# A retention, routing and GLU kernel: attention products turned round, first routing round without GpSimd arithmetic, TensorE rounds written out

## What is computed

```python
# retention over B=4 batches, H=8 heads, S=768 steps, D=64
state = gamma * state + k[t] (outer) v[t];   y[t] = q[t] @ state / sqrt(D)
x = y.transpose(0, 2, 1, 3).reshape(3072, 512)
# routing: 8 experts, 384 tokens each; all 3072*8 logits are taken in falling order,
# a token goes to the first expert that still has room
logits = x @ w_gate;  assigned = greedy(logits, cap=384)
out[e] = relu(x[e] @ w1[e]) @ w2[e]          # 512 -> 1024 -> 512
# gated unit on all tokens, d_ff = 1536
return (sigmoid(out @ w_gate2) * (out @ w_val)) @ w_out
```

## Time and profile before

| | us |
|---|---|
| three runs | 1206.94, 1212.17, 1213.2 (median 1212.17) |
| the profiled execution | 1207.1, its span 1205.4 |
| attention, to the first instruction of the search | 0 to 191.6 |
| first search and gather | 191.6 to 253.4 |
| eight rounds of work | 253.4 to 1194.2 |
| last copies and scatter | 1194.2 to 1205.4 |

### The profile page before, as it was taken

The page is one execution under the profiler, slowest core; times in us unless marked ns, Lnnn a source line. Parts: engine busy times, 40 slices in busy tenths (PEclk is TensorE's granted clock), DMA queues, the critical chain, the costliest instruction groups (busy, mean ns, idle before and its releaser), DMA issues.

```text
span 1205.4 us, 20115 instructions
## 1 busy us (share of the span) xinstructions
PE 1117.8 (93%) x7224; PEld 1032.8 (86%) x7224; DVE 573.7 (48%) x1423; ACT 339.7 (28%) x635; POOL 377.4 (31%) x365
## 2 busy tenths in 40 slices
PE   6999994169999999999999999999999999999996
PEld 6999993169889988998899889988998899899995
DVE  2343335865644564456345735572557255722111
ACT  2223222124123322332233223322331233223211
POOL 4432323245032513341234123322432143215200
PEclk9999996569999999999999999999999999999998
DMA  9878714223122211221132113111312131204100
GB/s 211 189 169 181 163 50 122 78 62 98 36 62 78 87 44 52 87 78 44 52 96 70 44 52 96 70 52 44 108 57 64 32 113 52 78 17 132 35 1 27
DMA packets 172925, 95.89 MB, mean 80 GB/s; under 512 B 80224, under 2 KB 158048, under 8 KB 172896
## 3 DMA queue, kind: packets, MB, share of 16 engines
q1 hardware_dynamic: 169056, 82.92, 26.2%
q0 software_dynamic: 3840, 12.59, 3.6%
HBM read 82.90 MB, written 12.58 MB: 79 GB/s over the span
## 4 chain that ended last, share of the span: by engine, by line
PE 68%; DVE 12%; issue 3%; ACT 1%; POOL 0%; DVEq 0%; POOLq 0%
PE bank L1103 18%; PE bank L1105 17%; PE bank L1104 17%; PE bank L1181 5%; PE bank L1183 5%; PE bank L1182 5%; DVE onehot L945 3%; DVE above L848 2%; DVE digit_f L868 1%; PE bank L1062 1%; PE bank L1098 1%; ACT ph L780 1%; PE bank L1070 1%; DVE pf L987 1%; DVE prefix L888 1%
## 5 line engine op out<-in xcount | busy, mean ns | idle before, releaser
L712 POOL TENSOR_TENSOR ring<-ring_raw,ring 128x512 fp32r<-128x512 f32 x192 | 247.4, 1296 | 456.2 <-ACT ring L760 451.9
L1103 PE MATMUL bank<-h2h,resident 128*128 128x384 f32 x768 | 263.3, 343 | 0.2
L1105 PE MATMUL bank<-h2h,resident 128*128 128x384 f32 x768 | 258.0, 336 | 0.0
L1104 PE MATMUL bank<-h2l,resident 128*128 128x384 f32 x768 | 257.6, 335 | 0.0
L987 DVE TENSOR_TENSOR pf<-bank,gate 128x384 f32<-128x384 f32 x96 | 53.2, 555 | 201.3 <-PE bank L1105 197.7
L1103 PEld LDWEIGHTS bank<-h2h,resident 128*128 128x128 f32 x768 | 144.4, 188 | 4.0 <-DVE h2l L978 0.4
L1104 PEld LDWEIGHTS bank<-h2l,resident 128*128 128x128 f32 x768 | 144.3, 188 | 3.2
L1105 PEld LDWEIGHTS bank<-h2h,resident 128*128 128x128 f32 x768 | 144.1, 188 | 0.0
L760 ACT ACTIVATE ring<-ring_raw 128x512 fp32r<-128x512 f32 x192 | 117.6, 623 | 70.6 <-DMA ring_raw<-in_moe_w_out_dram 40.9
L780 ACT ACTIVATE ph<-pf 128x384 fp32r<-128x384 f32 x96 | 50.4, 525 | 251.8 <-DVE pf L987 251.8
L776 ACT ACTIVATE gate<-bank 128x384 f32<-128x384 f32 x96 | 47.1, 491 | 212.0 <-PE bank L1105 212.0
(11 more groups left out here) (167 smaller groups left out, 1851.8 us busy)
## 6 DMA issues: line engine op xcount, KB each, us to landing
ring_raw<-in_moe_w_dram SPq DMA_DIRECT2D x128, 256.0 KB, 2.9
ring_raw<-in_moe_w_out_dram SPq DMA_DIRECT2D x64, 256.0 KB, 2.8
qraw<-in_q_dram SPq DMA_DIRECT2D x24, 256.0 KB, 3.6
kraw<-in_k_dram SPq DMA_DIRECT2D x24, 256.0 KB, 4.2
vraw<-in_v_dram SPq DMA_DIRECT2D x24, 256.0 KB, 4.7
xrows<-xrow SPq DMA_DIRECT2D x24, 256.0 KB, 2.2
resident_raw<-in_moe_w_gate_dram SPq DMA_DIRECT2D x12, 256.0 KB, 4.6
resident_raw<-in_moe_w_val_dram SPq DMA_DIRECT2D x12, 256.0 KB, 4.7
```

The costliest lines, as they stand in the source:

```text
L712: nc.gpsimd.tensor_tensor(ring[:, s, 1, :], ring_raw[s][:, :], ring[:, s, 0, :].bitcast(F32), ALU.subtract).then_inc(piece_lo, 1)
L1103: nc.tensor.matmul(ps, wh, xhi, start=start, stop=False)
L1104: nc.tensor.matmul(ps, wh, xlo, start=False, stop=False)
L1105: return nc.tensor.matmul(ps, wl, xhi, start=False, stop=stop)
```

## The change

It does six things.

- Attention on TensorE: y comes out transposed (`ps_y` holds features by tokens): `state` or `vraw` is the stationary operand with 64 columns, `qT` or `att` the moving one with 128, and the output goes to the half of the partitions that belongs to the head. The state's update is likewise one product a head, 64 columns of weights and 64 moving columns. The scores alternate between even and odd heads instead of four even ones and then four odd ones. `xTa` is now copied straight from `ps_y`, and the rows for HBM (`xrow`) from the transposed `ps_x`; the logits follow in the slot of those transposes, so there is one slot fewer.
- The first search: GpSimd no longer makes the 12 late low parts there, nor the first 8 of the ring. VectorE makes those 8 (`first_low`), four ahead of `x_low` and four behind it. The 12 late ones go into GpSimd's round 0, two after each of the pieces 16 to 21.
- GpSimd's round 0 stands ahead of its loop.
- TensorE's rounds are written out one after another, with no loop.
- `PART_GAP` is us(4).
- The last `out_products` counts each third (`rows_done`), and `out_rows` waits third by third.

```diff
-        DIGIT_GAP, LATE_GAP, PART_GAP = us(6.8), us(5), us(2)
+        DIGIT_GAP, LATE_GAP, PART_GAP = us(6.8), us(5), us(4)
...
# ScalarE, attention
-                        nc.scalar.activation(xTa[:, cc % 2, :, :], ps_x[:, :].rearrange("p (a t) -> p a t", a=KD),
-                                             ACT.Copy).then_inc(xT_ready, 1)
+                        nc.scalar.activation(xrow[:, cc, :], ps_x[:, :], ACT.Copy).then_inc(xrow_ready, 1)
...
-                        nc.scalar.activation(xrow[:, cc, :], ps_y[:, :], ACT.Copy, scale=SCALE).then_inc(xrow_ready, 1)
+                        nc.scalar.activation(xTa[:, cc % 2, :, :], ps_y[:, :].rearrange("p (a t) -> p a t", a=KD),
+                                             ACT.Copy, scale=SCALE).then_inc(xT_ready, 1)
...
# TensorE, attention
                         for a in range(KD):
-                            last = nc.tensor.transpose(ps_x[:, a * P:(a + 1) * P], xrow[:, cc, a * P:(a + 1) * P], ident[:, :])
+                            last = nc.tensor.transpose(ps_x[:, a * P:(a + 1) * P], xTa[:, cc % 2, a, :], ident[:, :])
...
                             if cc > 0:
-                                nc.tensor.matmul(ps_y[:, a * P:(a + 1) * P], qT[:, cc % 3, a, :], state[:, cc % 2, a, :],
-                                                 start=True, stop=False)
-                            for h in (2 * a, 2 * a + 1):
-                                last = nc.tensor.matmul(ps_y[:, h * D:(h + 1) * D], att[:, cc % 2, h, :], vraw[:, cc, h, :],
-                                                        start=cc == 0, stop=cc == 0 or h % 2 == 1)
+                                for half in range(2):
+                                    rows = slice(half * D, half * D + D)
+                                    nc.tensor.matmul(ps_y[rows, a * P:(a + 1) * P], state[:, cc % 2, a, rows], qT[:, cc % 3, a, :],
+                                                     start=True, stop=False)
+                            for half in range(2):
+                                rows = slice(half * D, half * D + D)
+                                last = nc.tensor.matmul(ps_y[rows, a * P:(a + 1) * P], vraw[:, cc, 2 * a + half, :],
+                                                        att[:, cc % 2, 2 * a + half, :], start=cc == 0, stop=True)
...
                             for a in range(NPAIR):
-                                last = nc.tensor.matmul(ps_u[:, a * P:(a + 1) * P],
-                                                        ks[:, cc, 2 * a:2 * a + 2, :].rearrange("p h d -> p (h d)"),
-                                                        vraw[:, cc, 2 * a:2 * a + 2, :].rearrange("p h d -> p (h d)"),
-                                                        start=True, stop=True)
+                                for half in range(2):
+                                    rows = slice(half * D, half * D + D)
+                                    last = nc.tensor.matmul(ps_u[rows, a * P + half * D:a * P + half * D + D],
+                                                            ks[:, cc, 2 * a + half, :], vraw[:, cc, 2 * a + half, :],
+                                                            start=True, stop=True)
...
-                        for half in range(2):
-                            rows = slice(half * D, half * D + D)
-                            if s is None or s - 2 >= 1:
-                                pe.wait_ge(att_ready, 2 * (u - 1) + half + 1)
-                            for a in range(NPAIR):
+                        if s is None or s - 2 >= 1:
+                            pe.wait_ge(att_ready, 2 * u)
+                        for a in range(NPAIR):
+                            for half in range(2):
+                                rows = slice(half * D, half * D + D)
                                 last = nc.tensor.matmul(ps_s[half][:, a * P:(a + 1) * P], kT[rows, cc % 2, a, :],
                                                         qT[rows, cc % 3, a, :], start=True, stop=True)
...
# GpSimd, second block
                     piece_low(i, n)
+                    if n >= 2 * RING:
+                        for k in late[:2]:
+                            late_low(k)
+                        late = late[2:]
...
-            for k in range(LATE):
-                late_low(k)
             gather(0)
-            for n in range(RING):
-                piece_low(0, n)
-            with pool.Fori(0, E - 1) as i:
-                one_round(i, True)
-            one_round(E - 1, False)
+            pool.wait_ge(piece_lo, RING)
+            one_round(0, True, list(range(LATE)))
+            with pool.Fori(1, E - 1) as i:
+                one_round(i, True, [])
+            one_round(E - 1, False, [])
...
# VectorE
+            def first_low(n):
+                dve.wait_ge(piece_hi, n + 1)
+                nc.vector.tensor_tensor(ring[:, n, 1, :], ring_raw[n][:, :], ring[:, n, 0, :].bitcast(F32),
+                                        ALU.subtract).then_inc(piece_lo, 1)
+
             def out_rows(i):
-                dve.wait_ge(out_done, KG * (i + 1))
                 for j in range(TT):
+                    dve.wait_ge(rows_done, TT * i + j + 1)
...
+            for n in range(RING // 2):
+                first_low(n)
             for a in range(KD):
                 x_low(0, a)
+            for n in range(RING // 2, RING):
+                first_low(n)
...
# TensorE, second block
-                        if j == TT - 1:
+                        if f == KG - 1:
+                            last.then_inc(rows_done, 1)
+                        elif j == TT - 1:
                             last.then_inc(out_done, 1)
...
-            with pe.Fori(0, E - 1) as i:
-                one_round(i, True)
-            one_round(E - 1, False)
+            for i in range(E):
+                one_round(i, i < E - 1)
```

More of the change, by code:

```diff
@@ L240, in retention_moe_glu_kernel @@
         out_done = sem("out_done")
+        rows_done = sem("rows_done")
         orow_ready = sem("orow_ready")
@@ L516, in body @@
                                                 ALU.mult).then_inc(qs_ready, 1)
-                    if alive(s, 5):
-                        bb, cc = unit(b, c, 5)
+                    if alive(s, 4):
+                        bb, cc = unit(b, c, 4)
                         u = bb * C + cc
@@ L548, in body @@
                                 causal[:, :].unsqueeze(1).to_broadcast([P, NPAIR, P]), ALU.mult).then_inc(att_ready, 1)
-                slots(dve, body, 0, U + 4)
+                slots(dve, body, 0, U + 3)
             @block.tensor
@@ L626, in body @@
                         pe.wait_ge(kT_ready, u + 1)
[L627 to L631 removed]
+                        if s is None or s - 2 >= 1:
[3 more added lines that the diff above has]
+                                rows = slice(half * D, half * D + D)
                                 last = nc.tensor.matmul(ps_s[half][:, a * P:(a + 1) * P], kT[rows, cc % 2, a, :],
                                                         qT[rows, cc % 3, a, :], start=True, stop=True)
[L634 to L636 removed]
+                                if a == NPAIR - 1:
+                                    last.then_inc(scores_done, 1)
+                slots(pe, body, 0, U + 3)
         block = ctx.enter_context(nc.Block())
@@ L725, in scatter, with one_round @@
                 pool.sem_inc(orow_free, 1)
-            def one_round(i, follows):
+            def one_round(i, follows, late):
                 gathered = not follows
```

26 lines of the change are left out of this document (10 added, 16 removed).

## The result

| | before | after |
|---|---|---|
| median of four runs | 1212.35 us | 1145.47 us |
| lowest and highest | 1206.94, 1213.2 | 1142.82, 1147.63 |
| profiled execution, its span | 1207.1, 1205.4 | 1147.63, 1145.9 |
| ratio of the times | | 0.9456 (95%: 0.9421 to 0.9491) |

The kernel is 5.4% faster. Split at the same events, the two profiled executions give this. The expert's rounds are measured from one set of x transposes to the next.

A forecast was written before the change was run, and what follows sets the result against it. TensorE's queue bounds attention, VectorE's chain the search, then dense TensorE with two waits a round. 29.1 + 14.3 - 2.5 + 11.3 + 1.4 = 53.6 us off 1207.1 or 1212.2 gives 1153.5 or 1158.6; forecast 1156, own range 1142 to 1166, overall 1140 to 1180.

The forecast's parts named there:

- Attention: First block, TensorE's queue: 1.24 us less a slot over 22 slots, 29.1 us in the sum, other ends included.
- y: Attention's output products: 32 instructions for 24, column halves side by side, 0.89 us gained a slot; one after another, 0.90 lost.
- update: State update in attention: 16 instructions of 64 by 64 for 8, taken as no change; range gain 0.45, loss 0.9.
- seams: Changes of how the array is cut in a slot: three instead of two, costing 0.20 us, between 0 and 0.4.
- The search: First search, GpSimd silent: comparisons faster, 7.3 us, and TensorE's first expert matmul no longer held by `digit_f`, 7.0; 14.3 us gained.
- Round 0: First expert round: 12 late GpSimd pieces slow VectorE's search there; 2.5 us lost, bounds 0 and 7.3.
- fourth rival: Expert rounds: TensorE's waits before L1089 and L1181 only move, and round 0 costs its 7.3 us; 1168 us, chance 0.10.
- The parts further apart: Expert rounds, PART_GAP at 4 us: 6.8 us of one-hot waits and 4.5 before L1181 go; 11.3, bounds 4 and 14.3.
- Loop and thirds: TensorE's written-out rounds and GpSimd's peeled round gain nothing; scatters at the end, started by thirds, gain 1.4 us.
- halves of columns don't overlap: Rival in attention's y: column halves run one after the other, +0.40 us a slot, total gain 15; 1194 us, chance 0.13.
- each change of half drains: Rival in attention: every switch between column halves in y and update costs 0.19 us, 97 lost; 1282 us, chance 0.04.
- loads come late: Rival in attention: later store and fuller DMA queues hold the slot at 6.6 us, 14 us lost; 1170 us, chance 0.08.

## Why the prediction came out right, and which terms were off

It said 1156 us, 1140 to 1180; the kernel takes 1145.5. The forecast, not a rival, is what happened, but the sum was 6 us too small by the profiled executions, and two of its terms erred in opposite directions.

**Attention** gave 40.0 us where the sum had 29.1. By the full slot, predicted 7.57 to 6.33 and measured 5.70:

| us a full slot | predicted | measured | from |
|---|---|---|---|
| scores | -0.55 | -0.55 | 1.64 to 1.09 |
| y | -0.89 | -0.99 | 2.68 to 1.69 |
| update | 0 (bound -0.45) | -0.42 | 1.09 to 0.67 |
| seams | +0.20 | +0.10 | 2.16 to 2.25 |

The mechanism was right for the scores and for y, whose halves do overlap, and one more seam came, at half its price. The mis-sized term is the update, and with it the cause that was taken to set a step. The prediction had the bound at the right place (0.45) and took the other value, arguing that loads of 128 columns cost 0.112 us with 64 or with 128 moving columns, so that the weights' columns set the step. In the runs 64 columns of weights take 0.11 us a pair with 128 moving columns (y) and 0.058 with 64 (the update, 16 loads in 0.60 us: in the trace its pairs start at 98.03, 98.14, 98.19, 98.25 and so on). Both old rows and new ones fit a step set by the larger of the two; that is a fit to four combinations, not a test. In the earlier trace rows the larger was 128 everywhere, so those rows could not tell one from the other; what would have was to ask which of the two numbers had ever been seen alone. The update's 0.42 us are worth 7.7 over the some 18 slots that have one, and with the cut kept the same from y on, no seam came between y and the update. The tenth in y and the tenth in the seams make 4.4 us more over 22 slots. That is 12.1 us; the sum was exceeded by 10.9, so 1.2 went at the two ends of attention. Of that 1.1 is a wait that the kernel before doesn't have, of TensorE for GpSimd's `ks` at 23.01 us.

**The search** gave 14.0 against 14.3. That comparisons go back to 1.03 us, that `digit_f` was held up and not slow, and that `first_low` hides behind `xh`, all came as worked out; the first expert matmul comes 47.8 us behind the search's start, 47.5 expected.

**Round 0** cost more than the 2.5 us taken. Alone, the change of the search lengthens it by 5.3 to 7.2 us (123.63 against 118.30 and 116.39 in kernels with the old search). In the kernel after it is 124.03 against the 115.24 of the gap alone, 8.8 us, and 6.5 in its other profiled execution (121.69). Without the half clock at the start of the round, which is a matter of the execution, it is 7.7 to 8.1 alone and 9.2 and 8.0 in the kernel after: above the upper bound of 7.3. Of these some 6 are waits, and 1.7 is each stretch at half clock behind them. This half of the fourth rival did happen. The step that failed is "TensorE waits only for what exceeds the gaps between due times": the comparisons exceed those gaps five times, for 5.3 us of waits, and behind the waits TensorE runs at half clock for a while, which no term had. The Trainium skill, page "SBUF — State Buffer", section "Who interferes with whom", says that such instructions contend with GpSimd, by which `p_low` was to be held up too and the cost to lie nearer the upper bound; the trace agrees (1.43 us against 0.56, and `h2l` with one operand in PSUM at 0.54 beside GpSimd), and it was the better guide to this term.

**The parts further apart**: 11.3 predicted, 10.2 in rounds 1 to 6 and 1 to 3 in round 0 measured alone. The one-hots' 6.8 went whole; of the 7.5 for `p_low`, 3.6 went instead of 4.5, and 0.57 us a round stayed instead of 0.4. The other half of the fourth rival, that these waits only move, is out, since none took their place.

**Loop and thirds** were right: nothing, and 11.17 to 9.81 us. The scatters start at 1136.25 and 1138.83 in the kernel after, and TensorE's last matmul at 1135.69: the first scatter no longer waits for the last product.

**The rivals.** That halves of columns don't overlap (1194) and that each change of half drains (1282) both fall with one row: four loads, of both halves, in 0.20 us. The Trainium skill, page "TensorE: Matmul & The Clock Gate", section "Part 3: Packing small matmuls — row/col tiling", ties the overlap of loads to a different row group; here the row group is the same (all 128 rows) and the measurement decides against it. That loads come late (1170) falls with the windows: 197 GB/s, 85% of the DMA engines' time, full slots of 5.70 us, and behind 20 us no wait of VectorE's `qs` or of TensorE on a DMA.

**The median** fell by 66.9 us, the profiled span by 59.5. The kernel before has times near 1206 and near 1211 us (15 runs on one chip: 1205.87 to 1212.46), and its profiled execution is one of the shorter; the prediction, midway between 1153.5 and 1158.6, had half of that. The last section has what lies between them.

**What adds up.** By medians the parts alone are 43.4, 11.6, 15.1 and 0, and 1.4 for the thirds, which weren't run alone: 71.5 against 66.9. By profiled executions with the same start of attention (1205.4 for the kernels of attention and gap, 1209.8, that of the written-out rounds, for the search) they are 39.7, 6.5, 12.9 and 1.4: 60.5 against 59.5. So the parts hardly touch each other.

**What stays open**: why TensorE is granted its full clock sooner in some executions; whether state products that use only the 64 rows of their own head, with other heads' beside them, would save part of y, since this wasn't tried.

## What to carry to other kernels

If an engine's own queue is the bound, ask for each run of its instructions which part of the array it uses, and put instructions for different parts next to each other, but keep the same cut from one step to the next: here order alone was worth 12.5 us in the scores and 28.4 in y, and each needless change of the cut 0.18. For a price that no row shows alone, list which of its two possible causes every row has at its maximum; the rows then tell that they can't decide, and the range has to carry it. Moving work to another engine's quiet stretch is not free if the two engines slow each other down: look for the slack of every instruction it will lie beside, and change the order of what waits before the amount. To price a wait, take the distance between the starts on both sides of it and subtract the usual one: the idle time listed was 0.57 us where 0.83 were lost.

## What the runs showed that wasn't expected

**One operation held up by many.** `digit_f` took 10.32 us for 0.33 us of work, because eight GpSimd pieces followed each other without a pause. It wasn't slowed by a factor: it got through when the row of pieces ended. All four profiled kernels with those eight pieces show it (10.32 or 10.33 us), and none of the nine without them. Why it waits for the whole row, while the comparisons beside the 12 late pieces get in between them (3.05 us for two), no run shows.

**A wait can cost once more, in clock.** After waits in round 0 TensorE runs at half speed for a while. Matmuls of the kernel after, timeline:

```profile
245.00 0.53 PE L1118 MATMUL bank<-h2h,resident 128*128 128x384 f32 x1
245.32 0.53 PE L1116 MATMUL bank<-h2h,resident 128*128 128x384 f32 x1
```

They start 0.32 us apart from 244.04 to 247.4, where the usual distance just before is 0.17. The windows of this time show the granted clock below 1.00, which it was from 210 to 240 us:

```profile
240.00:245.00 5.00, 3.16 (x19) 2.64 (x18) 3.04 (x4) 2.45 (x4) 5.00 (x5) 0.89 0.36 108
245.00:250.00 5.00, 5.00 (x27) 4.54 (x27) 2.09 (x4) 1.15 (x3) 5.00 (x5) 0.77 0.00 0
```

TensorE had been idle for 1.84 of 5 us and was then granted 1.2 instead of 2.4 GHz for some 3.4 us, in which it did half of what it could: 1.7 us lost with no wait to be seen. It happened twice in the profiled execution of the kernel after, the second time from 254.1 to 257.5. The other profiled execution of this kernel, whose round 0 took 121.69 us, has nearly the same waits (5.5 us) but a clock of 1.00 from 240 to 250 us and only one such stretch, 250.9 to 254.3. It also begins round 0 with 1.1 us at half clock where the first has 3.5. One stretch less is 1.7 us and the shorter beginning 1.2; the two rounds differ by 2.3. The four kernels with the old search, which have next to no waits on comparisons in round 0, show no such stretch in it; of the nine other profiled executions one shows none, seven show one and this one two. So the waits come first, but whether the clock falls behind them isn't the same each time.

**Two beginnings of attention.** The kernel before and the one with the rounds written out have the same attention, yet the search starts at 191.61 us in one profiled execution and at 197.36 in the other. The windows 20 to 30 us of the first,

```profile
20.00:30.00 10.00, 10.00 (x90) 9.64 (x90) 3.56 (x7) 2.77 (x5) 4.07 (x5) 1.00 1.25 257
```

and of the second:

```profile
20.00:30.00 10.00, 10.00 (x49) 9.55 (x49) 2.82 (x5) 1.79 (x3) 4.53 (x7) 1.00 1.25 258
```

TensorE is busy throughout in both and does 90 loads in the one, 49 in the other. Up to about 31 us each of its instructions takes twice as long in the second; the four loads of a transpose group take 0.87 instead of 0.47 us. The view's granted clock reads 1.00 in both, but that is no reading: the first clock record of the trace, at full clock, begins at 20.58 us in the one and at 30.75 in the other, and before its first record the view prints 1.00. So the second runs 10 us longer at what is by its rate the lower level. The two other kernels with the old attention fit: first record at 19.08 and search at 191.30 us for the gap, 31.89 and 197.43 for the search. That accounts for the 5 us between the two groups of times of the kernel before, though its slower group was never profiled. In the nine profiled executions of the new attention, whole or with a part taken back, the first record begins between 15.4 and 21.6 us, and the four runs of the new attention alone lie within 1.2 us. So it seems to begin in one way only, and that would be the greater part of the 7.4 us by which the medians differ more than the profiled executions. That wasn't tested, nor is it known what decides between the two beginnings.
